# Work moved from VectorE to GpSimd, reordered steps, and two transfers on other queues, in an attention and two-layer mixing kernel

## What is computed

```
k_sum = k.reshape(B, H, nb, 32, D).max(axis=3)
v_sum = v.reshape(B, H, nb, 32, D).mean(axis=3)
scores = [where(|i-j| < 16, q@k.T, -1e9), q@k_sum.T + log(32)] * scale
x = softmax(scores) @ [v, v_sum]               # B=2, H=8, S=768, D=64 -> x: 2 x 768 x 512
u = x + (relu(x.T @ w_tok1) @ w_tok2).T        # 768 -> 256 -> 768
x = u + relu(u @ w_ch1) @ w_ch2                # 512 -> 1536 -> 512
xn = (x - mean) / sqrt(var + 1e-6) * g_ln
out = x + relu(xn @ w2_ch1) @ w2_ch2           # 512 -> 2048 -> 512
```

## Time and profile before

| | before |
|---|---|
| median of 3 runs | 595.18 us (594.17 to 596.35) |
| profiled execution | 596.95 us, its span 595.2 us |
| TensorE busy | 575.4 us (97%) |
| weight loads of TensorE | 501.9 us (84%) |
| VectorE, ScalarE, GpSimd busy | 312.3, 228.9, 224.4 us |
| granted TensorE clock, mean | 0.993 |
| moved by transfers | 94.38 MB, mean 159 GB/s |

### The profile page before, as it was taken

One profiled execution on the slowest core, in us unless ns is written; L12 is line 12 of the kernel. 1 busy time (PEld: TensorE's weight loads), 2 busy tenths in 40 slices (PEclk: granted clock), 3 DMA queues, 4 the chain that ended last, 5 costly groups with the idle time before them and its releaser, 6 DMA issues.

```text
span 595.2 us, 8251 instructions
## 1 busy us (share of the span) xinstructions
PE 575.4 (97%) x2976; PEld 501.9 (84%) x2976; DVE 312.3 (52%) x668; ACT 228.9 (38%) x432; POOL 224.4 (38%) x208
## 2 busy tenths in 40 slices
PE   6889999997999999999999998999999999999997
PEld 2677888885889988898888987989888989899896
DVE  6476656487444345743445777433345644444443
ACT  3477664562333334343236323534325221212210
POOL 5356464215455568000317975344577100000000
PEclk9899999999999999999999999899999999999999
DMA  8877630065544374444414273445464334434602
GB/s 241 245 211 219 187 115 24 2 229 194 193 147 151 119 300 162 151 159 160 159 36 142 88 254 151 177 161 194 160 260 158 133 134 136 148 147 159 230 0 107
DMA packets 26913, 94.38 MB, mean 159 GB/s; under 512 B 7821, under 2 KB 8057, under 8 KB 23289
## 3 DMA queue, kind: packets, MB, share of 16 engines
q1 hardware_dynamic: 26320, 93.41, 45.1%
q10 hardware_dynamic: 552, 0.44, 0.3%
HBM read 64.42 MB, written 28.84 MB: 157 GB/s over the span
## 4 chain that ended last, share of the span: by engine, by line
PE 85%; DVE 7%; issue 3%; ACT 2%; DMA 2%; SPq 0%; POOL 0%; DVEq 0%; ACTq 0%; POOLq 0%
PE bank L557 81%; PE bank L660 1%; DMA v_turned<-v_t 1%; DVE neg_scores L1034 1%; DVE in_t L1016 1%; DVE down_w L1016 1%; ACT hidden L915 1%; PE bank L592 1%; PE bank L590 1%; PE bank L591 1%; DVE t_in L1076 1%; DVE bank L1099 1%; ACT probs L818 1%; DVE natural L1070 1%; DMA v_far<-v_mean 1%
## 5 line engine op out<-in xcount | busy, mean ns | idle before, releaser
L557 PE MATMUL bank<-down_w,hidden 128*128 128x512 f32 x1008 | 271.2, 397 | 1.3 <-DVE natural L1070 1.3
L557 PEld LDWEIGHTS bank<-down_w,hidden 128*128 128x128 f32 x1008 | 185.9, 189 | 27.2 <-issue 1.6
L915 ACT ACTIVATE hidden<-bank 128x384 fp32r<-128x384 f32 x112 | 55.0, 491 | 258.2 <-DVE bank L1099 185.6
L557 PE MATMUL bank<-in_t,up_even 128*128 128x384 f32 x588 | 120.7, 340 | 3.5 <-DVE hidden L1091 3.3
L557 PE MATMUL bank<-in_t,up_odd 128*128 128x384 f32 x588 | 119.4, 338 | 0.4 <-DVE hidden L1091 0.4
L557 PEld LDWEIGHTS bank<-in_t,up_even 128*128 128x128 f32 x588 | 106.5, 189 | 13.1 <-DVE hidden L1091 4.2
L557 PEld LDWEIGHTS bank<-in_t,up_odd 128*128 128x128 f32 x588 | 105.8, 188 | 9.5 <-DVE hidden L1091 0.8
L1091 DVE SCALAR_TENSOR_TENSOR hidden<-bank,hidden 128x384 fp32r<-128x384 f32 x112 | 62.4, 557 | 90.8 <-ACT hidden L915 90.7
L1143 DVE TENSOR_TENSOR u<-bank,p 128x384 f32<-128x384 f32 x28 | 15.6, 557 | 86.0 <-PE bank L557 86.0
L1099 DVE TENSOR_TENSOR bank<-bank,u 128x384 f32<-128x384 f32 x84 | 47.4, 564 | 19.5 <-PE bank L557 14.8
L1016 DVE TENSOR_TENSOR down_w<-raw_down,down_w 128x1024 fp32r<-128x1024 f32 x28 | 44.6, 1593 | 0.0
(11 more groups left out here) (92 smaller groups left out, 622.3 us busy)
## 6 DMA issues: line engine op xcount, KB each, us to landing
raw_down<-w_ch SPq DMA_DIRECT2D x28, 512.0 KB, 3.3
up_kept<-up_even SPq DMA_DIRECT2D x7, 1792.0 KB, 8.2
up_kept<-up_odd SPq DMA_DIRECT2D x7, 1792.0 KB, 8.2
up_even<-up_kept SPq DMA_DIRECT2D x7, 1792.0 KB, 7.5
up_odd<-up_kept SPq DMA_DIRECT2D x7, 1792.0 KB, 7.1
raw_up<-w_ch SPq DMA_DIRECT2D x14, 512.0 KB, 4.5
k_sb<-k_w SPq DMA_DIRECT2D x16, 273.0 KB, 4.2
v_own<-v_w SPq DMA_DIRECT2D x8, 390.0 KB, 3.3
```

Of the source, the lines that this page charges most:

```text
L557: return nc.tensor.matmul(dst, lhs, rhs, start=start, stop=stop, skip_group_check=True)
L915: nc.scalar.activation(hidden[:, q % 2, f, 0, h * HN:(h + 1) * HN], src, ACT.Relu).then_inc(hid_high, 1)
```

## The change

- **Transfers.** The mask is loaded by SP behind the first queries and no longer by ScalarE. The means of head pair 0 are sent by ScalarE's queue right behind its copy of them; for all others SP sends as before.
- **Token weights.** `tok_low_part` moves from VectorE to GpSimd, between the two `split_x` of a head pair.
- **Into the feed-forward.** TensorE turns the last input tile behind one `mix_hidden(1, 1, ...)` and no longer behind three. The low part of input 6 moves from VectorE to GpSimd. The down weights of pair 0 are rounded by ScalarE before input 5, and VectorE subtracts before pair 0 and no longer inside it.
- **GpSimd in pairs that make weights** waits for VectorE's `low_down(q)` before `low_sums(q + 1)` (not in the last pair of a group).
- **Layer norm.** VectorE keeps the reciprocal (`row_inverse`); six operations on 128x6 numbers go to GpSimd, behind its `low_sums`. Statistics, ScalarE's square root and its six scalings are placed anew in pairs 6 to 8 and 13 to 15.
- **Output additions.** `add_out` for tiles 1 to 5 is placed about one step later in pairs 6, 12 and 20.
- The spare tile `room` shrinks from 608 to 512 numbers for each partition.

```diff
...
+        def send_means(queue, r):
+            i = r % 2
+            queue.wait_ge(mean_copied, r + 1)
+            if r >= 2:
+                queue.wait_ge(pv_done, NT * (r - 1))
+            else:
+                queue.wait_ge(far_init, r + 1)
...
             load_k(0)
             load_q(0)
+            sp.dma_start(mask_sb[:], mask).then_inc(ld_mask, 16)
...
-            send_means(0)
             load_v(1)
...
+            def tok_low_part(k):
+                pool.wait_ge(tok_high, k + 1)
+                nc.gpsimd.tensor_tensor(tok_w[:, 1, k, :], tok_stage[:], tok_w[:, 0, k, :].bitcast(F32), ALU.subtract
...
+            def row_scales(ln):
+                r, tt = rstd, nc.gpsimd.tensor_tensor
+                pool.wait_ge(inverse, ln + 1)
+                tt(r[:, 1], r[:, 0], r[:, 0], ALU.mult).then_inc(newton, 1)
...
                     split_x(2 * r)
+                    if r < TOK_CH:
+                        tok_low_part(r)
                     split_x(2 * r + 1)
...
                 if making:
                     low_up(q + 1)
+                if q == 0:
+                    low_first(6)
+                if making and j < PAIRS_OF[g] - 1:
+                    pool.wait_ge(down_low, q + 1)
                 if making:
                     low_sums(q + 1)
+                if SCALE_AT.get(g) == j:
+                    row_scales(g - 1)
...
-            for t in range(GT):
+            mix_hidden(1, 1, 0, score_bank[0])
+            first_tile(NT - 1)
+            for t in range(1, GT):
                 mix_hidden(1, 1, t, score_bank[0])
-            first_tile(NT - 1)
...
                 if q == 0:
                     high_input(0, 4)
+                    high_down(0)
                     high_input(0, 5)
...
+                if scaled:
+                    normed(g - 1, 2)
+                    normed(g - 1, 3)
...
+                if scaled:
+                    normed(g - 1, 4)
+                    normed(g - 1, 5)
...
+                if scaling and g == 2:
+                    deviation(1)
...
+                if scaling and g == 1:
+                    deviation(0)
...
+                if scaling:
+                    normed(g - 1, 0)
+                    normed(g - 1, 1)
...
-            act.dma_start(mask_sb[:], mask).then_inc(ld_mask, 16)
...
             copy_means(0, mix_bank[0:NSUM, mean_at])
+            send_means(act, 0)
...
-                low_down(q)
                 if q == 0:
                     add_mixed(1, 2, o_bank[0])
-                    low_first(6)
+                else:
+                    low_down(q)
...
                 if opening:
-                    add_out(g - 1, 2)
-                    if g == 1:
-                        row_stats(0, 0)
-                if scaling:
-                    row_scales(g - 1)
+                    add_out(g - 1, 1)
...
+                if g == 2 and j == 2:
+                    row_inverse(1)
...
                 add_c(q, 0, 4, u3)
+                if opening:
+                    add_out(g - 1, 2)
...
+                if middle:
+                    row_inverse(0)
                 low_hidden(q, 2, product_bank(q, 5)[:, 0:HN])
...
-                if r < TOK_CH and t == 4:
-                    tok_low_part(r)
...
             sum_first(3, blk(1, 0), t_in[:, 1])
+            low_down(0)
             for q in range(NQ):
                 pair(q)
```

More of the change, by code:

```diff
@@ L282, in batch_bank @@
             return up_bank[(7 * q + 7 + k) % 2]
+        def send_means(queue, r):
[5 more added lines that the diff above has]
+                queue.wait_ge(far_init, r + 1)
+            for h in range(2):
+                at = SUM_ROW[h]
+                queue.dma_start(v_far[at:at + NSUM, i, :, 1 + h * D:1 + (h + 1) * D],
+                                v_mean[:, i, h * D:(h + 1) * D].rearrange("p (t n) -> p t n", t=1)
+                                .broadcast_to([NSUM, NT, D])).then_inc(ld_mean[i], 16)
         block = ctx.enter_context(nc.Block())
@@ L705, in up @@
                 use[0] += 1
-                if q == 0:
+                if q == 0 and i < 6:
                     pe.wait_ge(in_low, i + 1)
+                elif q == 0:
+                    pe.wait_ge(first_low_pool, 1)
                 elif j == 0:
@@ L921, in pair @@
                 scaling = SCALE_AT.get(g) == j
+                scaled = j and SCALE_AT.get(g) == j - 1
                 act.wait_ge(up_done, 7 * q + 1)
@@ L1139, in pair @@
                 opening = g > 0 and j == 0
-                scaling = SCALE_AT.get(g) == j
+                middle = g == 1 and j == 1
+                behind = g == 2 and j == 1
                 dve.wait_ge(up_done, 7 * q + 2)
@@ L1182, in pair @@
                     add_mixed(1, 3, o_bank[1])
+                if opening and g == 1:
+                    row_stats(0, 2)
+                add_c(q, 1, 5, u3)
                 if opening:
                     add_out(g - 1, 3)
-                    if g == 1:
-                        row_stats(0, 1)
-                if g == 2 and j == 1:
-                    row_stats(1, 3)
-                add_c(q, 1, 5, u3)
+                if behind:
+                    row_stats(1, 4)
+                if middle:
+                    row_inverse(0)
                 low_hidden(q, 2, product_bank(q, 5)[:, 0:HN])
@@ L1204, in pair @@
                     add_out(g - 1, 5)
-                    if g == 1:
-                        row_stats(0, 3)
-                if g == 2 and j == 1:
-                    row_stats(1, 5)
+                if behind:
                     row_moments(1)
```

108 lines of the change are left out of this document (50 added, 58 removed).

## The result

The changed kernel takes 593.37 us (median of 20 runs, 590.02 to 595.55) against 596.13 us before (20 runs, 594.17 to 599.45): a ratio of 0.9946, interval 0.9928 to 0.9965, a gain of 3.2 us (1.7 to 4.3). The forecast was a gain of 9.9 us. Its sign was right; the time lies above the range.

What follows compares the result with a forecast made beforehand. The prediction took TensorE's idle holes and low-clock stretches as the bound; 3.3 (attention) + 0.4 (start) + 2.2 (feed-forward) + 0.4 (pair 7) + 3.6 (pair 14) = 9.9 us off 595.18 us, forecasting 585.2 us, range 582.2 to 588.6 us.

Steps and rivals of the forecast that it cites:

- What bounds the kernel: Whole kernel: TensorE, busy 575.4 of 595.1 us; only its 19.7 us standing still and low-clock work can be won.
- Start: TensorE's wait for the first means at 17.09 us: gain 0.4 us, between 0.2 lost and 0.9 gained.
- rival (a): More goes: clock stays at 2.4 GHz after the 17 us stall, or collisions at 131 us miss; 582.0 us, chance 0.22.
- The mask: At the start: moving its 309 KB load to SP's queue, behind the queries, changes nothing.
- Attention: First four head pairs: token weights' low part leaves VectorE for GpSimd, gaining 3.3 us, bounds 2.5 to 3.7.
- Rival (b): Attention: GpSimd becomes the bound, key-maxima copies 1 us late in three head pairs; 588.0 us, chance 0.17.
- Into the feed-forward: 121 to 147 us: work taken off VectorE or done earlier gains 2.2 us, bounds 1.5 to 3.9.
- the short ratio: Near 131 us: alternative price of 0.4 us for each VectorE-GpSimd meeting, making the feed-forward term 2.9 us.
- -3.38 + 1.22: Into the feed-forward: pair 0's down-weight subtraction, 3.38 us in its old place, takes 1.22 us before pair 0.
- Pair 7: Later statistics and output additions moved into gaps remove a 0.41 us stall: gain 0.4 us.
- Pair 14: 363 to 372 us: VectorE freed earlier, 1.87 us stall gone and clock kept; gain 3.6 us, bounds 1.9 to 3.7.
- The spare tile: Making the spare tile smaller moves addresses only and gains nothing.

Runs made afterwards that it cites:

- e2_loads_held: Changed kernel, means still sent by ScalarE, but SP waits for their landing before issuing head pair 1's values and later loads; ratio to before 0.9887, 590.0 us.
- e3_before_act: Kernel before the change with only the first send of the means moved to ScalarE's queue; ratio to before 1.0129, 604.3 us.
- e4_sp_mask_act: As e1_sp_sends with the mask loaded by ScalarE again, so only the engines' work differs from the kernel before; ratio 0.9857, 587.49 us.
- e6_turned_first: As e1_sp_sends with turned values and token weights issued ahead of head pair 2's keys and queries; ratio to before 0.9836, 587.42 us.
- e1_sp_sends: Changed kernel with one thing undone: SP sends the first means again, ahead of head pair 1's values; ratio to before 0.9846, 587.75 us.
- y2_input6_dve: As e1_sp_sends with input 6's low part on VectorE again; run once, 29.16 us from tile 47 to the first down product.
- x3_down0_back: As e1_sp_sends with pair 0's down weights made inside pair 0 again; run once, 27.34 us from tile 47 to the first down product.
- x1_no_pool_wait: As e1_sp_sends without GpSimd's wait for VectorE's down weights before its low sums; run once, pair 14 takes 15.69 us.
- y1_room_608: As e1_sp_sends with the spare tile at 608 numbers again; run once, 443.86 us from the first down product to the end.
- e5: As e1_sp_sends, but SP sends the means ahead of the queries of head pair 1; ratio to before 0.9853, 587.91 us.
- e7: Against e6_turned_first, all first transfers ordered by need: turned values before the mask, means before head pair 1's queries; ratio to before 0.9829, 587.34 us.
- e8_turned_early: As e7 with each later head pair's turned values issued one step earlier; ratio to before 0.9829, 586.10 us.

## Why the prediction came out as it did

**What bounds the kernel: right.** TensorE's holes were nearly the whole story (the addresses, below, were the rest), and from tile 24 to tile 47, where it had none, nothing moved (55.51 and 55.54 us).

**Start: wrong, and this is the miss.** The forecast took 0.4 us of gain between bounds of 0.2 us lost and 0.9 us gained; the profile has 3.9 us lost up to tile 0 and 0.7 us behind it at the low clock, the repeated profile 6.2 and 1.4 us. The failed step is the bound. Both ends came from the landings of 2.4 to 3.5 us, and every one of those transfers stood in SP's own queue, ahead of the loads that SP issued later. The text noted that SP's loads would "follow at once and share the engines" and named the skill's rule that the queues interleave, and then priced neither: SP now issues 2178 KB (values, keys and queries, turned values, token weights) next to two small sends of 36 KB, and the bound on the loss had to be the time of that backlog, by my estimate some 9 us at the 250 GB/s that the trace shows. The three profiles with the same two sends waited 4.1, 6.3 and 6.9 us more than before, all within it. The Trainium skill (DMA: Bandwidth & Descriptors, "Issuing engines are not separate DMA queues") says that transfers run on the same 16 engines and interleave whichever engine issues them. The runs agree as far as they go: e2_loads_held brings the wait back to 3.6 us. Its further words, that issuing from several engines only saves time of issue, leave out what is measured here, a loss of 1.3% (e3_before_act). The old order had protected the means: SP stood still at them, so its later loads stayed out of the way. Also wrong was that the clock would do as before: the low clock covered 4.8 us of TensorE's work and 5.3 us of the stall itself, where it had covered 3.4 us of work. The length of a stall does not tell it alone. After 2.3 us the clock did not fall in e4_sp_mask_act, which is one half of rival (a), and it fell after 1.8 us in e6_turned_first.

**The mask: right**, nothing that the runs can tell (e4_sp_mask_act).

**Attention: right in size, with luck.** 3.3 us forecast, 3.32 us measured from tile 6 to tile 24. The reckoning of GpSimd was nearly right: its two copies start 3.1 and 3.6 us behind the first tile of the head pair and end at 3.9 us (forecast near 3.6), with 0.2 us or less lost:

```profile
42.49 1.82 POOL L464 TENSOR_TENSOR tok_w<-tok_stage,tok_w 128x768 fp32r<-128x768 f32 x1
...
43.05 0.39 PE L596 MATMUL bank<-v_far,probs_t 108*128 108x130 f32 x2
...
46.15 0.28 POOL L429 COPY k_sb<-k_sb 64x120 f32<-64x120 f32 x1 [0.19 <-POOL x_split L457]
46.39 0.39 PE L596 MATMUL bank<-v_far,probs_t 108*128 108x130 f32 x2
46.63 0.28 POOL L429 COPY k_sb<-k_sb 64x120 f32<-64x120 f32 x1 [0.20 <-issue]
...
48.18 0.39 PE L596 MATMUL bank<-v_far,probs_t 108*128 108x130 f32 x2
```

But with SP's loads in the old order the full 3.3 us are seen only where the start was late, most likely because that gives the transfers time. When SP sends in the old order and VectorE is rid of the token weights, the stretch takes 30.2 to 32.2 us in five profiles, e1_sp_sends with 31.17 us among them, a gain of 0.8 to 2.7 us (and 33.8 us in a sixth, y2_input6_dve, where the clock fell once more). Rival (b), GpSimd's copies late, holds in part: late turned values start the chain, and GpSimd's added 1.8 us lie in it.

**Into the feed-forward: right in size, wrong in its terms.** 2.2 us forecast, 2.38 us measured. The prediction's own working gives 2.1 us (139.46 to 137.4), and its lower bound of 1.5 us does not come out of waits of 2 us each, which would leave nothing of the 3.7 us. The collisions are the ones that the text described: input 4 takes 2.10 us (forecast 0.95 + 1.15) and input 5 1.51 us (0.95 + 0.45), and each ends 0.8 us after GpSimd's operation has ended; the short ratio of 0.4 us for each is refuted.

```profile
130.59 1.23 DVE L1067 TENSOR_TENSOR down_w<-raw_down,down_w 128x1024 fp32r<-128x1024 f32 x1
...
132.24 1.85 POOL L487 TENSOR_TENSOR up_odd<-raw_up,up_odd 128x768 fp32r<-128x768 f32 x1 [20.99 <-ACT up_odd L936]
...
132.80 2.10 DVE L1067 TENSOR_TENSOR in_t<-t_in,in_t 128x768 fp32r<-128x768 f32 x1
134.16 2.42 POOL L516 TENSOR_TENSOR in_t<-raw_in,in_t 128x768 fp32r<-128x768 f32 x1
...
135.89 1.51 DVE L1067 TENSOR_TENSOR in_t<-t_in,in_t 128x768 fp32r<-128x768 f32 x1
```

The Trainium skill (SBUF — State Buffer, "Who interferes with whom") calls what VectorE and GpSimd share an exclusive lock, and a VectorE instruction with two inputs in SBUF contends for it; the trace agrees. But the terms "-3.38 + 1.22" for the down weights are worth nothing as a move (x3_down0_back): GpSimd's wait shortens them in their old place, and in the new one they bring about the two collisions. Input 6, set at 0.95 us, is worth 1.70 us (y2_input6_dve), since it also holds GpSimd's low sums back from input 5. What the earlier turning gives was not tried alone.

**Pair 7: right and small.** 0.4 us forecast; the pair went from 16.43 to 15.69 us, the 0.41 us stall is gone, 0.06 us are the addresses', and some 0.27 us of the rest the prediction had not counted.

**Pair 14: right in size, half right in cause.** 3.6 us forecast, 3.8 us measured (19.51 to 15.69 us). In the changed kernel VectorE was ready at 363.4 us, before the product that it then waits for:

```profile
362.07 1.21 DVE L1067 TENSOR_TENSOR down_w<-raw_down,down_w 128x1024 fp32r<-128x1024 f32 x1
363.21 0.18 DVE L1169 RECIPROCAL rstd<-dev 128x6 f32<-128x6 f32 x1
364.03 0.56 DVE L1217 TENSOR_TENSOR u<-bank,u 128x384 f32<-128x384 f32 x1 [0.65 <-PE bank L596]
...
365.91 0.19 POOL L522 TENSOR_TENSOR rstd<-rstd 128x6 f32<-128x6 f32 x1
```

GpSimd's six small operations took 1.6 us, not 2. Its wait for the down weights was not needed in this pair (x1_no_pool_wait).

**The spare tile: wrong.** "Addresses only: nothing" was 1.3 us of gain (y1_room_608).

**Sum.** Of the profiles: 3.32 + 2.38 + 0.74 + 3.82, and some 1.2 us for the addresses, less 4.61 us, is 6.8 us. Without the one send on ScalarE's queue the kernel gains 1.54% (e1_sp_sends), 9.2 us of 596.13 us, against 9.9 us forecast. But 1.3 us of these are the addresses', which the forecast put at nothing: the terms that it did name come to 7.9 us.

## What to carry to other kernels

A queue that stands still at a wait also keeps its later loads out of the way of a small urgent transfer. Before such a transfer is moved to another queue, add up what the first queue will then issue, and take that backlog as the bound on the loss; durations of transfers that stood ahead of those loads tell nothing about it. And after a stall at the start is shortened, look at what comes next: with three of the four orders tried here (e5, e6, e7) tile 24 came at most 0.3 us earlier than in e1_sp_sends, since a late transfer one or two head pairs on, or a longer stretch at the low clock, took back what the start had given. One profile for each order is too little to price a gain of 1 us: those of one and the same order differ by up to 3.5 us at tile 24.

## What the runs showed of the hardware that I had not expected

- The granted clock did not follow the length of TensorE's stall: after 2.3 us of waiting at the start it was at 1.2 GHz for 0, 3.4 or 6.8 us (e4_sp_mask_act, e5_means_before_q1, e8_turned_early), with work at half speed for that time.
- Two sends of 144 pieces of 256 bytes each on ScalarE's queue were waited for 7.3 to 10.2 us when SP issued 2178 KB of loads beside them, 3.6 us when these were held back, and sends of 24 pieces as long (9.1 us) as those of 144.
- Moving the feed-forward's tiles by 384 bytes in each partition made a pair of 42 up and 36 down products 0.06 us faster, 15.75 to 15.69 us, in every pair without turns. Why was not tried.
- GpSimd takes 0.19 to 0.23 us for an operation on 128x6 numbers, where VectorE took 0.17 to 0.60 us for the five that did the same work.
